# The turn between two transform stages: through DRAM, or from SBUF to SBUF

## The reference

```python
X = np.fft.rfft(x, axis=1)
y = np.fft.irfft(X * (filt_r + 1j * filt_i)[None], n=3008, axis=1)
t = y.reshape(6016, 256)
xn = t / np.sqrt(np.mean(t * t, axis=-1, keepdims=True) + 1e-6) * rms_g
t = (silu(xn @ w_gate) * (xn @ w_val)) @ w_out      # 256 -> 1536 -> 256
h = np.maximum(t @ w_in2, 0)                        # 256 -> 2048
out = (s * h * h + b) @ w_out2                      # 2048 -> 256
```

## Time and profile before

| | us |
|---|---|
| median of 3 runs | 1401.77 |
| span of the profiled execution | 1402.1 |
| PE busy in it | 1304.6 (93%) |
| DVE, ACT busy | 700.7, 569.2 |
| first matmul of step 1, of step 2 | 11.20, 148.64 |
| last product of VectorE in the transform | 208.53 |

### The profile page before, as it was taken

How to read it: one execution, slowest core, us unless ns; L and a number is a source line. 1 busy time by engine, 2 the same in 40 slices (tenths; PEclk the granted TensorE clock), 3 DMA queues, 4 the chain that set the end, 5 groups by cost and what they waited for, 6 DMA issues and landing times.

```text
span 1402.1 us, 21932 instructions
## 1 busy us (share of the span) xinstructions
PE 1304.6 (93%) x7948; PEld 1226.3 (87%) x7948; DVE 700.7 (50%) x1157; ACT 569.2 (41%) x1147; POOL 141.2 (10%) x146
## 2 busy tenths in 40 slices
PE   4444879999999999999999999999999999999998
PEld 1101428999999999999999999999999999999998
DVE  0001686554544455545445446655555555555554
ACT  0001454333333333333333335555545554555454
POOL 0000346111011111111011102000000000000000
PEclk9999999999999999999999999999999999999999
DMA  1116995000000000000000100000000000000000
GB/s 49 53 54 194 262 307 176 12 12 12 1 12 11 11 11 11 11 11 11 5 6 0 60 1 1 12 12 12 12 11 11 11 11 11 11 11 11 11 12 23
DMA packets 33978, 51.77 MB, mean 37 GB/s; under 512 B 3632, under 2 KB 27568, under 8 KB 33680
## 3 DMA queue, kind: packets, MB, share of 16 engines
q1 hardware_dynamic: 33936, 51.22, 12.0%
HBM read 32.46 MB, written 18.74 MB: 37 GB/s over the span
## 4 chain that ended last, share of the span: by engine, by line
PE 86%; SPq 8%; DMA 3%; DVE 2%; ACT 1%; POOL 0%; issue 0%; ACTq 0%; DVEq 0%
PE bank L415 21%; PE bank L416 20%; PE bank L417 20%; SPq L242 7%; PE bank L503 7%; PE bank L502 6%; PE bank L504 6%; PE bank L397 2%; DMA m_ring<-per_j 1%; PE bank L359 1%; PE bank L384 1%; DMA by_r<-u_ring 1%; PE bank L369 1%; DMA v<-by_r 1%; SPq L243 1%; SPq L244 0%
## 5 line engine op out<-in xcount | busy, mean ns | idle before, releaser
L774 DVE TENSOR_TENSOR h<-bank,act 128x376 f32<-128x376 f32 x192 | 104.6, 545 | 305.4 <-PE bank L417 297.2
L800 DVE SCALAR_TENSOR_TENSOR h<-act,sc 128x376 f32<-128x376 f32 x256 | 159.6, 624 | 195.2 <-ACT act L617 189.9
L571 ACT ACTIVATE act<-bank 128x376 f32<-128x376 f32 x192 | 93.1, 485 | 370.1 <-PE bank L417 370.0
L617 ACT ACTIVATE act<-bank 128x376 f32<-128x376 f32 x256 | 124.6, 487 | 226.8 <-PE bank L417 226.2
L503 PE MATMUL bank<-out_lo,h_hi 128*128 128x256 f32 (+1 forms) x768 | 216.0, 281 | 0.0
L502 PE MATMUL bank<-out_hi,h_hi 128*128 128x256 f32 (+1 forms) x768 | 215.2, 280 | 0.0
L504 PE MATMUL bank<-out_hi,h_lo 128*128 128x256 f32 (+1 forms) x768 | 215.2, 280 | 0.0
L415 PE MATMUL bank<-xn_hi,in_hi 128*128 128x376 f32 x512 | 171.3, 335 | 0.2 <-issue 0.2
L416 PE MATMUL bank<-xn_lo,in_hi 128*128 128x376 f32 x512 | 170.9, 334 | 0.0
L417 PE MATMUL bank<-xn_hi,in_lo 128*128 128x376 f32 x512 | 170.5, 333 | 0.0
L806 DVE SCALAR_TENSOR_TENSOR h_lo<-h,bi,h_hi 128x376 fp32r<-128x376 f32 x256 | 157.6, 616 | 0.2 <-ACT h_hi L626 0.2
(11 more groups left out here) (87 smaller groups left out, 2202.5 us busy)
## 6 DMA issues: line engine op xcount, KB each, us to landing
by_r<-u_ring SPq DMA_DIRECT2D x32, 192.0 KB, 3.5
v<-by_r SPq DMA_DIRECT2D x12, 512.0 KB, 11.1
z_ring<-by_j SPq DMA_DIRECT2D x16, 384.0 KB, 3.5
x_all<-x SPq DMA_DIRECT2D x16, 376.0 KB
by_j<-v SPq DMA_DIRECT2D x22, 256.0 KB, 5.6
out<-staged SPq DMA_DIRECT2D x32, 128.0 KB, 2.1
f_ring<-filt SPq DMA_DIRECT2D x12, 256.0 KB, 5.5
in_raw<-w_in SPq DMA_DIRECT2D x1, 2048.0 KB, 14.7
```

The lines of the kernel that those rows point to most:

```text
L617: nc.scalar.activation(act[:, c % 2], bank[c % 4][:, 0:TILE], ACT.Relu).then_inc(relu_done, 1)
L774: nc.vector.tensor_tensor(h[:, c % 2], bank[2 * (c % 2) + 1][:, 0:TILE], act[:, c % 2], ALU.mult).then_inc(hmul_done, 1)
L800: nc.vector.scalar_tensor_tensor(out=h[:, c % 2], in0=act[:, c % 2], scalar=sc2[:], in1=act[:, c % 2], op0=ALU.mult, op1=ALU.mult).then_in ...
```

## The change

The tensor `by_r` goes. After copying chunk i, ScalarE issues the DMAs of chunk i - 1 from its own queue: one for each of the 4 r and each c, from 48 partitions of `u_ring` (1 KB each) straight into one partition of `v` (48 KB). A chunk's slot counts 8 DMAs in place of 2. TensorE waits for all of them once, behind the dummy matmuls, in place of a wait for each pair of j. SyncE issues `load_j(0)` to `load_j(3)` right behind the small tables, and the later ones four pairs ahead.

```diff
+PER_CHUNK = 16 * 2 * RC
...
-        v_in = [sem(f"v_in{i}") for i in range(NJ // JG)]
...
-            for i in range(NRC):
-                sp.wait_ge(u_act, i + 1)
-                sp.wait_ge(u_dve, i + 1)
-                for c in range(2):
-                    sp.dma_start(by_r[c, i * RC:(i + 1) * RC].rearrange("r jb d -> jb r d"),
-                                 u_ring[c * BATCH * NJ:(c + 1) * BATCH * NJ, i % UR]).then_inc(u_out[i % UR], 16)
-
-            load_j(0)
-            for q in u_out:
-                sp.wait_ge(q, 16 * 2 * NRC // UR)
-            for g in range(NJ // JG):
-                sp.dma_start(v[:, g * JG:(g + 1) * JG],
-                             by_r.rearrange("c r (j b) d -> (c r) j b d", b=BATCH)[:, g * JG:(g + 1) * JG]
-                             ).then_inc(v_in[g], 16)
-
-                if g in (0, 1, 2):
-                    load_j(g + 1)
-                if g in (6, 8, 10):
-                    load_j(g // 2 + 1)
+            for g in range(JRING // JG):
+                load_j(g)
...
-                if 2 <= g < NJ // JG - 5:
-                    load_j(g + 5)
+                if g < NJ // JG - JRING // JG:
+                    load_j(g + JRING // JG)
...
             def step2(j):
                 pe.wait_ge(m_full, j // JG + 1)
-                pe.wait_ge(v_in[j // JG], 16)
...
             keep_warm(7, 34)
+            for q in u_out:
+                pe.wait_ge(q, PER_CHUNK * NRC // UR)
             step2(0)
...
         def _(a):
+            def turn(i):
+
+                a.wait_ge(u_act, i + 1)
+                a.wait_ge(u_dve, i + 1)
+                for k in range(RC):
+                    for c in range(2):
+                        row = c * NR + i * RC + k
+                        a.dma_start(v[row:row + 1].rearrange("p j b d -> p (j b) d"),
+                                    u_ring[c * BATCH * NJ:(c + 1) * BATCH * NJ, i % UR, k]).then_inc(u_out[i % UR], 16)
+
             for i in range(NRC):
                 a.wait_ge(s1_mm, i + 1)
                 if i >= UR:
-                    a.wait_ge(u_out[i % UR], 32 * (i // UR))
+                    a.wait_ge(u_out[i % UR], PER_CHUNK * (i // UR))
                 nc.scalar.copy(u_ring[:, i % UR, 0:2], ...).then_inc(u_act, 1)
+                if i:
+                    turn(i - 1)
+            turn(NRC - 1)
```

More of the change, by code:

```diff
@@ L90, in spectrum_tables, with build @@
             step4.astype(np.float32), signs.astype(np.float32), rows)
-def build(nc, by_r, by_j, x, filt, step1, per_j, step4, signs, w_gate, w_val, w_out, rms_g, w_in2, w_out2, scale2, bias2, out):
+def build(nc, by_j, x, filt, step1, per_j, step4, signs, w_gate, w_val, w_out, rms_g, w_in2, w_out2, scale2, bias2, out):
     with ExitStack() as ctx:
@@ L698, in _ @@
                 if i >= UR:
-                    dve.wait_ge(u_out[i % UR], 32 * (i // UR))
+                    dve.wait_ge(u_out[i % UR], PER_CHUNK * (i // UR))
                 nc.vector.tensor_copy(u_ring[:, i % UR, 2:4],
@@ L934 @@
     out = nc.dram_tensor("out", (TOKENS, DIM), F32, kind="ExternalOutput").ap()
-    by_r = nc.dram_tensor("by_r", (2, NR, NJ * BATCH, DIM), F32, kind="Internal").ap()
     by_j = nc.dram_tensor("by_j", (2, NJ, BATCH, NR, DIM), F32, kind="Internal").ap()
-    build(nc, by_r, by_j, *args, out)
+    build(nc, by_j, *args, out)
     r = run_bass_kernel_spmd(nc, [arrays], core_ids=[0])
```

## The result

The changed kernel takes 1498.32 us (median of 4 runs, 1496.87 to 1501.9) where the kernel before takes 1401.41 (median of 4, measured beside it): a ratio of 1.070 (95% interval 1.068 to 1.072). It is 97 us slower.

A forecast was written before the change was run, and what follows sets the result against it. Dense-layer TensorE matmuls fill most of the chain; the change touches only the front, held by x's arrival. Step 2's start moves from 148.6 to 220.5 us (+71.9), less 4.7: +67.2 on 1401.77, forecast 1469, 8-in-10 range 1395 to 1550.

The forecast's parts named there:

- x is carried by two engines and holds the front: Front, until about 121 us: two of sixteen DMA engines carry x without rest, one chunk per 7.33 us.
- One partition as the destination: Turn DMAs into v: one partition takes 26.5 GB/s, so 7.4 us per chunk with two rows side by side.
- The Trainium skill's account of the ports: Turn writes into v: four neighbouring partitions share a port of about 27 GB/s; a chunk needs 7.2 to 14.5 us.
- x's engines lose that time: x's arrival: its engines also sit in turn pieces, so the period becomes 12.8 us (11.0 to 14.7), 5.5 more.
- Issuing: ScalarE's queue: 0.45 us per turn DMA (0.35 to 0.65), 3.6 us per chunk, hidden while x arrives.
- The last two turns: Behind chunk 15's copy: two turns still to move, 14.8 us, then 3 us landing, before step 2 starts.
- The 4.7 us in steps 2 and 3: VectorE's products: its 4.7 us wait for TensorE goes, with v's reads gone and loads issued earlier; bounds 0 and 5.3.
- The signs: Expected in the trace: matmuls 11 to 15 us apart, share far above 0.13 at 75 GB/s, VectorE idle under 1 us.
- 1 (x loses nothing): Front: one partition takes the full rate and x's engines lend time free; -16.9 us, 1385; chance 0.13.
- 2 (shared engine time only): Front: one partition takes the full rate, x loses 1.4 us per chunk; +2.7 us, 1405; chance 0.13.
- 3 (ScalarE's issues held behind SyncE's): Queues: both pass one place, so 113 turn DMAs remain after 113 us; 1416; chance 0.09.
- 4 (one row after another): Turn: rows strictly in sequence, 14.8 us per chunk, 1512; if x's time is added too, 1614; chance 0.12.

The follow-up runs named there:

- before_x: The kernel before the change with each x load cut in two, partitions 0 to 79 and 80 to 93: 1306.58 us, ratio 0.930 to the uncut one.
- spread: The changed kernel with each turn DMA's 48 pieces written to 48 partitions of v in place of one, same bytes and queue: 1412.66 us.
- third: The changed kernel with each turn DMA cut to 16 of its 48 pieces, still 128 DMAs: 1404.07 us.
- turn_sp: The changed kernel with the turn's 128 DMAs on SyncE's queue behind x and the tables: 1485.28 us.
- c_outer: The changed kernel with the turn's two loops swapped, a chunk's four rows of c=0 first, then c=1; same bytes to the same places: 1564.85 us.
- port1: The changed kernel with a chunk's eight rows all sent to one group, four neighbouring partitions and those 32 higher: 1580.26 us.
- ports8: The changed kernel with a chunk's four r sent four partitions apart, so its eight rows lie in eight groups of partitions: 1495.88 us.
- spread_x: The changed kernel with turn DMAs written to 48 partitions of v each and the x loads cut at partition 80: 1352.85 us.

## Why the prediction was right, point by point

The forecast was 1469, 29 below the result. The side, the limit (one partition as the destination) and the place where it costs (x's arrival) were right. How x loses the time was not as the prediction had it, and that 12.8 us came near 14.2 is in part luck: it is the middle between a value for turn-taking that does not happen and an upper end that nothing in the trace before could show. Its steps:

- *x is carried by two engines and holds the front.* Shown, by before_x more than by anything else: with the 94 rows cut into 80 and 14 the front shrinks by 94.8 us.
- *One partition as the destination.* This was the unknown that decided, taken by its upper end, 26.5 GB/s per row with two rows side by side. Shown: spread (other destination), with third (fewer bytes) and turn_sp (turn alone, 62 GB/s at a share of 1.17) beside it. 7.4 us per chunk was taken; 6.4 was measured without x. "Two rows side by side" is so only while neighbours in the queue lie in different groups: c_outer costs 4.6 us per chunk more, port1 5.3.
- *The Trainium skill's account of the ports* (SBUF, State Buffer; Door 1: The DMA port swizzle) fits port1 and c_outer: partitions 4i to 4i+3 and those 32 higher behave as one way in, those 64 higher as another. The estimate of 7.2 us per chunk at best that the prediction worked out from its figure was a little too high (6.4 measured), and counting ports over a chunk, as I first did, is not what decides; ports8 shows it.
- *x's engines lose that time.* Taken as 12.8 us between starts, from 11.0 to 14.7; measured 14.2. This is the mis-sized term: 1.4 us x 14 chunks = 20 us. (Chunk 15's own gap is longer, 16.2 us, so the whole miss up to it is 219.7 - 198.2 = 21.5 us.) The upper end, "one excludes the other", was nearly exact in size. Of the 6.9 us added per chunk 1.1 are engine time (spread) and 5.8 the pile (14.2 - 8.4). The step behind the number was wrong: x's engines do not sit in the turn's pieces, and x's pieces do not pass in turn with them. On x's two engines the turn's 48 pieces start after the pile, from 32.1 us on, and what stretches is x's own packets, from 0.159 to 0.93 us.
- *Issuing.* 0.45 us taken, 0.61 in the median measured (5.0 us for eight, 0.63 each). Hidden beside x in the changed kernel; on the path in spread (11.1 us for the last sixteen).
- *The last two turns.* 14.8 + 3 taken behind the last copy, 20 measured (224.1 to 244.2 us).
- *The 4.7 us in steps 2 and 3.* Failed in size: the stage takes 244.19 to 303.37, 59.2 us against 60.6, a gain of 1.4. VectorE keeps 2.3 us of idle before L709, most of it behind a load_j that now stands behind the weights in SyncE's queue, and its first product starts later. In this row of that queue the ring's load is issued only after 1.5 MB of down_raw:

```profile
283.95 1.21 SPq L284 DMA_DIRECT2D down_raw<-w_out  x1
285.45 2.72 SPq L257 DMA_DIRECT2D f_ring<-filt  x1
288.20 0.60 SPq L258 DMA_DIRECT2D m_ring<-per_j  x1
```

  and the chain in order of time has the landing that it waits for:

```profile
288.20 7.56 DMA m_ring<-per_j
```

- *The rest carried over.* From the last product to the end 1192.4 us, before 1192.8.
- *The signs.* Spacing between 11 and 15 us, the wait for u_ring gone, the rest as before: these came. The DMA share beside x rose less than said (0.23, at 55 GB/s in place of 75, from 32 to 46 us), and VectorE's idle time did not fall below 1 us.

The sum as measured, in us: +98.5 (x of chunk 15) - 2.9 (behind it) - 1.4 (stage) - 0.4 = +93.8, against the spans' +93.7.

The rivals: 1 (x loses nothing) is refuted by the spacing. 2 (shared engine time only) is what spread is, and its 8.7 us and 1405 stand beside 8.4 and 1412.66; its missing 7 us are the slower issuing and the stage. 3 (ScalarE's issues held behind SyncE's) is refuted by 5.0 us per eight issues while SyncE's queue stood full. 4 (one row after another) is what c_outer comes near: 1564.85.

Left open: that about two neighbouring DMAs overlap is inferred from ports8, port1 and c_outer; why not three or four was not tested. Each engine has three pieces of a DMA; a run with one or six was not made at full bytes. Nor do the runs tell where x's slow packets wait, in their engines or on the way into the partitions.

## What to carry to other kernels

Look at what a DMA's destination looks like at one moment, not only at its bytes. Sixteen engines that all write one partition at a time were here about as slow as the two that carried x (62 against 53 GB/s), the profile calls them busy all the while once their queue is full (share 1.17), and another load's packets took six to ten times as long beside them. Before a DRAM round trip is taken out, see whether the direct way has this shape; here 12.6 MB of traffic through DRAM were much cheaper than 6.3 MB within SBUF. And count the issues: 128 small DMAs at 0.63 us each are 80 us, whatever their destination (spread_x). Read the DMA share beside GB/s first: a share of 0.13 at 53 GB/s said that x was on two engines, and cutting its 94 rows into 80 and 14 was worth more than anything done to the turn.

## What the runs showed of the hardware that I had not expected

- The order of two loops of DMA issues, with the same bytes to the same places, is worth 67 us (1564.85 against 1498.32).
- DMA writes that have been issued, and whose pieces have started, still hold others back: x moves at 10 GB/s after the turn's last issue, and its packets that start from 28.5 to 29.9 us still take 0.94 to 0.98 us.
- The granted clock in the front differs between profiles: 0.5 to 0.6 in the slices of ports8's and third's front, 0.9 and more in most of the changed kernel's. Step 1's groups of matmuls show 3.73 us in each, and the times agree with the spacing by DMA, so I draw nothing from it.
- The same 376 KB of x take 7.33 us, or about a fifth of it (1.46 us at the 263 GB/s that before_x moves from 5 to 20 us), by whether they go as one DMA of 94 rows or as two of 80 and 14. The Trainium skill (DMA: Bandwidth & Descriptors, How many engines (k)) has the rule: a DMA runs on the largest number of engines up to 16 that divides its slowest dimension, which makes 2 for 94 rows, 16 for 80 and 14 for 14. For the 94 rows this case agrees (0.13 of sixteen engines), and it shows the size: 94.8 us of the front.
